# Router logits of chunk 4 as VectorE dot products from y in place, instead of TensorE transposes and matmuls

## What is computed

```python
def _moe2_ref(x, modality_id, w_gate, modality_bias, w1, w2):
    logits = x @ w_gate + modality_bias[modality_id]      # 2304 x 8
    e_idx = np.argmax(logits, axis=1)                     # one expert per token
    logits_s = logits - logits.max(-1, keepdims=True)
    probs = np.exp(logits_s)
    probs /= probs.sum(-1, keepdims=True) + 1e-09
    gate_w = probs[np.arange(N), e_idx]
    for e in range(E):
        mask = e_idx == e
        h = np.maximum(x[mask] @ w1[e], 0.0)
        out[mask] = gate_w[mask, None] * (h @ w2[e])
```

## Time and profile before

| | us |
|---|---|
| runs of the kernel before: median (lowest to highest) | 873.07 (871.36 to 874.25) |
| the profiled execution: span from first to last instruction | 870.5 |
| TensorE busy | 857.1 (98%) |
| VectorE busy | 520.7 (60%) |
| ScalarE busy | 374.4 (43%) |
| GpSimd busy | 328.4 (38%) |
| block 3 of the last chunk | 532.28 to 539.86 |

### The profile page before, as it was taken

The page is one execution under the profiler, slowest core; times in us unless marked ns, Lnnn a source line. Parts: engine busy times, 40 slices in busy tenths (PEclk is TensorE's granted clock), DMA queues, the critical chain, the costliest instruction groups (busy, mean ns, idle before and its releaser), DMA issues.

```text
span 870.5 us, 15612 instructions
## 1 busy us (share of the span) xinstructions
PE 857.1 (98%) x5233; PEld 736.4 (85%) x5242; DVE 520.7 (60%) x1401; ACT 374.4 (43%) x945; POOL 328.4 (38%) x372
## 2 busy tenths in 40 slices
PE   8999999999999999999999999999999999999997
PEld 5678898888888888899999999988888888888885
DVE  6985555333453335449778763883877457666663
ACT  6966313545464455443321132243356235554442
POOL 3736762344323443356335333170043221222211
PEclk9999999999999999999999999999999999999999
DMA  9983212212223210242121121526265645555531
GB/s 191 289 212 88 61 48 65 84 55 78 53 60 112 52 38 27 71 157 74 42 93 61 61 73 37 210 81 254 97 205 206 241 144 191 184 213 182 192 128 39
DMA packets 77517, 103.40 MB, mean 119 GB/s; under 512 B 38973, under 2 KB 43069, under 8 KB 77312
## 3 DMA queue, kind: packets, MB, share of 16 engines
q1 hardware_dynamic: 73760, 91.16, 33.9%
q0 software_dynamic: 3680, 11.28, 3.7%
HBM read 92.98 MB, written 10.22 MB: 119 GB/s over the span
## 4 chain that ended last, share of the span: by engine, by line
PE 89%; DVE 8%; issue 1%; ACT 1%; POOL 1%; DMA 1%; SPq 0%; DVEq 0%; POOLq 0%; ACTq 0%
PE ps L1243 32%; PE ps L1282 16%; PE ps L1805 13%; PE ps L1790 13%; PE ps L1174 3%; PE ps L1203 2%; PE ps L1815 2%; PE ps L1184 2%; PE ps L1150 2%; PE ps L660 1%; DVE sm L1520 1%; DVE w_lo L2041 1%; DMA qk<-in_k 1%; PE ps L1312 1%; DVE h_lo L1600 1%
## 5 line engine op out<-in xcount | busy, mean ns | idle before, releaser
L1035 POOL TENSOR_TENSOR sm<-sm,rinv 72x288 f32<-72x288 f32 (+1 forms) x51 | 45.5, 893 | 174.2 <-DVE rinv L1531 174.1
L1067 POOL TENSOR_TENSOR out_lo<-out_raw,out_hi 128x512 fp32r<-128x512 f32 x72 | 101.8, 1414 | 5.8
L1589 DVE SCALAR_TENSOR_TENSOR h<-h,ps 128x384 f32<-128x384 f32 x72 | 39.8, 553 | 104.2 <-ACT h L1437 103.3
L1243 PE MATMUL ps<-x_hi,val_hi 128*128 128x384 f32 x288 | 101.1, 351 | 0.0
L1243 PE MATMUL ps<-x_hi,gate_hi 128*128 128x384 f32 x288 | 100.5, 349 | 0.4 <-DVE h L1589 0.4
L1065 POOL CAST out_hi<-out_raw 128x512 fp32r<-128x512 f32 x72 | 50.0, 694 | 135.0 <-DMA out_raw<-in_moe_w_out 135.0
L1441 ACT ACTIVATE h_hi<-h 128x384 fp32r<-128x384 f32 x72 | 37.8, 525 | 138.7 <-DVE h L1595 138.7
L1243 PE MATMUL ps<-x_hi,gate_lo 128*128 128x384 f32 x288 | 97.1, 337 | 0.0
L1243 PE MATMUL ps<-x_hi,val_lo 128*128 128x384 f32 x288 | 96.6, 336 | 0.0
L1243 PE MATMUL ps<-x_lo,val_hi 128*128 128x384 f32 x288 | 96.5, 335 | 0.0
L1243 PE MATMUL ps<-x_lo,gate_hi 128*128 128x384 f32 x288 | 93.9, 336 | 0.0
(11 more groups left out here) (278 smaller groups left out, 1947.5 us busy)
## 6 DMA issues: line engine op xcount, KB each, us to landing
w_raw<-in_moe_w SPq DMA_DIRECT2D x72, 512.0 KB, 4.9
out_raw<-in_moe_w_out SPq DMA_DIRECT2D x72, 256.0 KB, 2.6
x_rows<-y_tiles SPq DMA_DIRECT2D x18, 256.0 KB, 2.7
early_w_raw<-in_moe_w SPq DMA_DIRECT2D x8, 512.0 KB, 7.6
gate_raw<-in_moe_w_gate SPq DMA_DIRECT2D x4, 768.0 KB, 9.1
val_raw<-in_moe_w_val SPq DMA_DIRECT2D x4, 768.0 KB, 10.5
qk<-in_q SPq DMA_DIRECT2D x8, 288.0 KB
qk<-in_k SPq DMA_DIRECT2D x8, 288.0 KB
```

The lines of the kernel that those rows point to most:

```text
L1035: pool.tensor_tensor(s3, s3, rinv[0:n, i, :].unsqueeze(2).to_broadcast([n, 4, c]), ALU.mult).then_inc(s_no, 1)
L1067: pool.tensor_tensor(ol[i][:, :], o_raw[i][:, :], oh[i][:, :].bitcast(f32), ALU.subtract).then_inc(s_ol, 1)
L1243: mm = pe.matmul(ps[:, bank, 0:CH], w[:, i, kk, cols], x[:, kk, :], start=(m == 0), stop=(m == n - 1))
L1589: dve.scalar_tensor_tensor(out=hf[n % 2][:, :], in0=hf[n % 2][:, :], scalar=1.0, in1=ps[:, 0, 0:CH], op0=ALU.add, op1=ALU.mult).then_inc(s ...
```

## The change

The logits of chunk 4's three tiles are no longer made by TensorE. VectorE makes them as 24 more dots, which read `ys` in place, without a reload: tile 12, 13 and 14 stand at places 9, 10 and 11 of the list of dotted tiles (`DOTTED_TILES`). They are spread over the 21 ticks from the second half of block 0's gate third to block 3's value third of chunk 5 (`FRESH_TICKS`): 6 dots in block 0, 7 in block 1, 7 in block 2, 4 in block 3. The nine reloaded tiles now end with chunk 4 (`AGAIN_TICKS`), so their dots and their reload DMAs move forward by up to four and six ticks. `evac_y` of chunk 5 waits for the dots instead of the transposes. `one_hot` now waits for 12 dotted tiles and 3 by TensorE.

```diff
--- before.py
+++ after.py
@@ -114,16 +114,14 @@
 
 SS = {0: 16, **{c + 1: at(c, 9, 2) for c in range(NC - 1)}}
 SPREAD = {c: s + (2 if c == 0 else 6) for c, s in SS.items()}
-Y_TILE = {(NC - 2, t): at(NC - 1, 1 + t, 0) for t in range(TT)}
-LOGITS = {k: s + 2 for k, s in Y_TILE.items()}
+Y_TILE, LOGITS = {}, {}
 SS_AT = by_tick((c, s) for c, s in SS.items())
 SPREAD_AT = by_tick((c, s) for c, s in SPREAD.items())
 NORMED = {(c, kk): SPREAD[c] + 1 + (min(kk, 2) if c else 0) for c in SPREAD for kk in range(KT)}
 NORMED_AT = by_tick((k, s) for k, s in sorted(NORMED.items()))
 BANK7 = [x for s in range(TICKS) for x in
          [("p", j) for j in TURN_AT.get(s, [])] + [("o", j) for j in PV_AT.get(s, []) if s >= EARLY]
-         + [("ss", c) for c in SS_AT.get(s, []) if c] + [("rb", c) for c in SPREAD_AT.get(s, []) if c]
-         + [("y", k) for k, x in Y_TILE.items() if x == s] + [("lg", k) for k, x in LOGITS.items() if x == s]]
+         + [("ss", c) for c in SS_AT.get(s, []) if c] + [("rb", c) for c in SPREAD_AT.get(s, []) if c]]
 BEFORE7 = {x: BANK7[n - 1] if n else None for n, x in enumerate(BANK7)}
 
 
@@ -134,19 +132,24 @@
         Y_TILE[c, t], LOGITS[c, t] = free[t], free[t + 1]
 Y_AT = by_tick((k, Y_TILE[k]) for k in sorted(Y_TILE))
 LOGITS_AT = by_tick((k, LOGITS[k]) for k in sorted(LOGITS))
-TURNED_Y = [sum(x < s for k, x in Y_TILE.items() if k[0] < NC - 2) for s in range(TICKS + 1)]
-TURNED_LOGITS = [sum(x < s for k, x in LOGITS.items() if k[0] < NC - 2) for s in range(TICKS + 1)]
-
-
-
-DOTTED = TT * (NC - 3)
+TURNED_Y = [sum(x < s for x in Y_TILE.values()) for s in range(TICKS + 1)]
+TURNED_LOGITS = [sum(x < s for x in LOGITS.values()) for s in range(TICKS + 1)]
+
+
+
+RELOADED = TT * (NC - 3)
+DOTTED_TILES = [*range(RELOADED), *range(TT * (NC - 2), TT * (NC - 1))]
+DOTTED = len(DOTTED_TILES)
 ROUTER = at(NC - 3, 3, 1)
 PAUSE = (SPAN - 6, 0)
-DOT_TICKS = [s for s in range(at(NC - 3, 5, 0), at(NC - 1, 1, 0, 1)) if PAUSE[1] < (s - EARLY) % SPAN < PAUSE[0]]
-DOT = {(i, e): DOT_TICKS[(E * i + e) * len(DOT_TICKS) // (E * DOTTED)] for i in range(DOTTED) for e in range(E)}
+AGAIN_TICKS = [s for s in range(at(NC - 3, 5, 0), at(NC - 1, 0, 0)) if PAUSE[1] < (s - EARLY) % SPAN < PAUSE[0]]
+FRESH_TICKS = range(at(NC - 1, 0, 0, 1), at(NC - 1, 3, 2))
+DOT = {(i, e): (AGAIN_TICKS[(E * i + e) * len(AGAIN_TICKS) // (E * RELOADED)] if i < RELOADED else
+                FRESH_TICKS[(E * (i - RELOADED) + e) * len(FRESH_TICKS) // (E * (DOTTED - RELOADED))])
+       for i in range(DOTTED) for e in range(E)}
 DOT_AT = by_tick((k, s) for k, s in DOT.items())
 DOTTED_AT = by_tick((i, DOT[i, E - 1] + 1) for i in range(DOTTED))
-RELOAD_AT = by_tick((i, DOT[i, 0] - 8) for i in range(DOTTED))
+RELOAD_AT = by_tick((i, DOT[i, 0] - 8) for i in range(RELOADED))
 BY_EXPERT_AT = by_tick((e, DOT[0, e] - 1) for e in range(E))
 
 
@@ -510,13 +513,13 @@
 
         def turned(c, t):
 
-            return TT * c + t - DOTTED
+            return TT * c + t - RELOADED
 
         def y_bank(c):
-            return 7 if c == NC - 2 else 6
+            return 6
 
         def logits_bank(c):
-            return 7 if c == NC - 2 else 5
+            return 5
 
         def ss_bank(c):
             return 7 if c else 0
@@ -1102,12 +1105,8 @@
                     pe.wait_ge(s_oe, before[1] + 1)
                 elif before[0] == "ss":
                     pe.wait_ge(s_nv, before[1] + 1)
-                elif before[0] == "rb":
+                else:
                     pe.wait_ge(s_rc, before[1])
-                elif before[0] == "y":
-                    pe.wait_ge(s_yte, turned(*before[1]) + 1)
-                else:
-                    pe.wait_ge(s_le, turned(*before[1]) + 1)
 
             def residues():
                 pe.wait_ge(s_ms, 2)
@@ -1285,13 +1284,10 @@
                     mm.then_inc(s_y, 1)
 
             def y_bank_free(what, c, t):
-                if c == NC - 2:
-                    bank_7_free((what, (c, t)))
-                else:
-                    s = (Y_TILE if what == "y" else LOGITS)[c, t]
-                    scores_read(s)
-                    pe.wait_ge(s_qe, TURNED_QK[s])
-                    side_free(s)
+                s = (Y_TILE if what == "y" else LOGITS)[c, t]
+                scores_read(s)
+                pe.wait_ge(s_qe, TURNED_QK[s])
+                side_free(s)
 
             def turn_y(c, t):
 
@@ -1445,8 +1441,10 @@
                 act.wait_ge(s_y, FT * c + FT)
                 if c:
                     act.wait_ge(s_x2, 16 * TT * c)
-                    if turned(c, 0) > 0:
-                        act.wait_ge(s_yt, turned(c, 0))
+                    if c >= NC - 2:
+                        act.wait_ge(s_yt, TT)
+                    if c == NC - 1:
+                        act.wait_ge(s_dot, E * DOTTED)
                 act.activation(ys[:, :, :], ps[:, 2:2 + TT, :], ACT.Copy).then_inc(s_ye, 1)
 
             def evac_yT(c, t):
@@ -1602,15 +1600,19 @@
 
             def dot(i, e):
 
-                if e == 0:
+                again = i < RELOADED
+                if e == 0 and again:
                     dve.wait_ge(s_ya[i % 3], 16 * (i // 3) + 16)
+                if e == 0 and i == RELOADED:
+                    dve.wait_ge(s_ye, NC - 1)
                 if i == 0:
                     dve.wait_ge(s_rwe, e + 1)
                 if E * i + e:
                     dve.wait_ge(s_dot, E * i + e)
                 if e == 0 and i >= 2:
                     dve.wait_ge(s_ld, i - 1)
-                dve.tensor_tensor_reduce(out=unread[:, :], in0=y_again[i % 3][:, :], in1=rw_of[e][:, :], scale=1.0,
+                y = y_again[i % 3][:, :] if again else ys[:, DOTTED_TILES[i] % TT, :]
+                dve.tensor_tensor_reduce(out=unread[:, :], in0=y, in1=rw_of[e][:, :], scale=1.0,
                                          scalar=0.0, op0=ALU.mult, op1=ALU.add,
                                          accum_out=dots[:, i % 2, e:e + 1]).then_inc(s_dot, 1)
 
@@ -1618,7 +1620,8 @@
                 if i == 0:
                     dve.wait_ge(s_bu, 6)
                 dve.wait_ge(s_dot, E * i + E)
-                dve.tensor_tensor(logit[:, i, :], dots[:, i % 2, :], bias_t[:, i, :], ALU.add).then_inc(s_ld, 1)
+                n = DOTTED_TILES[i]
+                dve.tensor_tensor(logit[:, n, :], dots[:, i % 2, :], bias_t[:, n, :], ALU.add).then_inc(s_ld, 1)
 
             def add_bias(c, t):
                 i = TT * c + t
```

## The result

Changed kernel: median 878.28 us (876.34 to 880.20, 9 runs); kernel before beside it on the same chip: 871.46 us (869.37 to 874.86, 9 runs). The ratio is 1.0067, 95% interval 1.0048 to 1.0086: slower by about 5.8 us (the medians lie 6.8 us apart), where 3.5 us was forecast. Its profiled execution took 880.04 us, its span is 878.3 us.

A forecast was written before the change was run, and what follows sets the result against it. TensorE held 89% of the chain of waits; the change would make VectorE the bound up to hot_b. -4.0 (TensorE) + 7.9 (TensorE waiting for VectorE) - 0.4 = +3.5 us on 873.07: 876.6 us, range 871.8 to 879.8.

The forecast's parts named there:

- Taken from TensorE: Chunk 4's three tiles: transposes, logits and a longer product leave TensorE, 1.32 us per tile, 4.0 us saved on the path.
- Given to VectorE: Chunk 5, blocks 0 to 3: 24 dots, 17.0 us, make VectorE the bound; hot_b at 540.9 us even with GpSimd silent.
- GpSimd's part: GpSimd's w_out splits beside VectorE's work in blocks 1 to 4 of chunk 5: four times 1.2 us, together 4.8 us.
- Start: First dot of VectorE's queue, after ScalarE's ys and held by GpSimd's out_lo: gets going at about 515.4 us.
- What comes after: After the one-hot: VectorE runs on without pause, so TensorE's wait at 573 us goes, -0.4 us.
- The third rival: TensorE's clock falls in the wait before early_counts, costing 1.7 us more: 878.3 us, chance 0.23.
- Moved: Four dots of tile 8 go into chunk 4, reloaded dots up to four ticks forward, covered by VectorE's gaps: 0 us.

The follow-up runs named there:

- e5: Changed kernel with only chunk 4's first tile on VectorE, its dots in blocks 1 and 2, reloaded dots not moved: ratio 0.9966 to the kernel before.
- e10: The kernel e5 run once more on another occasion, no new edit: ratio 0.9981 to the kernel before.
- e2: Changed kernel with GpSimd's subtraction for w_out's low part cut to 8 columns in blocks 1 to 4 of chunk 5: ratio 1.0040 to the kernel before.
- e3: Changed kernel with 20 matmuls of 384 columns into an unused bank put ahead of early_counts, filling the wait: ratio 1.0048 to the kernel before.
- e7: Changed kernel without the move: reloaded dots keep their old ticks, 24 new dots stand in blocks 1 to 3 of chunk 5: ratio 1.0075.
- e1: Kernel before with only the reloaded dots moved to end with chunk 4; chunk 4's own tiles stay with TensorE: ratio 1.0029.
- e4: Changed kernel with early_counts moved to the middle of block 4's down product, 3.1 us of TensorE work later: ratio 1.0044 to the kernel before.
- e9: e1 with GpSimd's subtraction cut to 8 columns for three blocks around the end of chunk 4, TensorE's matmul count kept: ratio 1.0004.
- e6: Changed kernel with two of chunk 4's tiles on VectorE, reloaded dots not moved, early_counts later: ratio 0.9997 to the kernel before.

## Why the prediction was right, and where it was not

The forecast was 876.6 us with a range of 871.8 to 879.8 and 0.67 on slower; 878.28 us was measured. That the time lies only 1.7 us off is in part luck: the forecast was built on a median before of 873.07 us, and beside the changed kernel that kernel ran at 871.46. The step forecast was 3.5 us, and the step measured 5.8 by the ratio. The direction and the cause, VectorE late with `hot_b`, were right. Step by step:

- **"Taken from TensorE", 4.0 us: right.** e5 and e10 got 1.2 to 1.4 us for one tile. In the changed kernel chunk 5 shows none of it, because VectorE became the bound, as "Given to VectorE" said.
- **"GpSimd's part", 4.8 us: right**, 4.84 us by the rows, and e2 got back the 2.6 us of it that its edit removed. Two of the four places were other instructions than dots: h_split, and `pick` in the one-hot.
- **"Start", 515.4 us: 0.8 us too late, counted from the mark.** I had GpSimd hold the first dot. In the changed kernel its subtraction ended at 518.16 us, before the copy of y did at 518.69 us, since the copy came 1.7 us later and the split did not. Another 0.5 us of the sum was too much: without GpSimd's part, VectorE took 25.0 us from the first dot to the end of `hot_b`, and I had added up 25.5. So `hot_b` was late by 2.6 us, and not by 3.9.
- **"What comes after", -0.4 us: right**, 0.6 us came back.
- **The third rival, the clock, had 0.23, and it came**, at 1.5 us where 1.7 us was the price. e3 shows it by taking the wait away. It should have been in the forecast: a wait of about 4 us in TensorE's work was forecast, and the trace held an example of the clock at 0.66 without any such wait. The Trainium skill ("TensorE: Matmul & The Clock Gate", "HAM oscillation") says that a long gap sends the clock back; here the traces agree, with waits of 3.67 us (changed kernel), 3.75 (e2), and 2.74 and 3.81 (e7). Behind the 1.60 us at the end of chunk 4 the clock stayed at 1.00.
- **"Moved", 0 us: wrong, +1.7 us in this profile, 2.5 us by e1's ratio.** This is the step that failed. I read one gap of 1.46 us in the middle of chunk 4, called it the cover, and let the dots move into the last blocks of the chunk, where VectorE has the roots, the diagonals and the normalising of the next chunk as well, and where each dot could meet a split. My own, from that very place, showed it with no idle time and dots of 1.00 and 1.29 us. I had used them for chunk 5 and not for the place that they came from. The way that the dots move was too short as well: by the tables it is up to six ticks, and thirteen for the last four of tile 8, not "up to four". e1, e4, e7 and e9 show what stands in place of the 0: with the move, the normalising for the next chunk comes so late that it meets a split, and when the subtraction comes first TensorE waits 1.3 to 1.6 us for the h_split behind it.

In chunk 5 two errors cancel, which is luck: 2.5 - 0.6 + 1.5 = 3.4 us, where 3.9 - 0.4 = 3.5 was forecast. What the profiled execution lies above the forecast step is chunk 4 (1.7 us) and 0.3 us after chunk 5.

The cost of the move differs between executions: 1.27 to 1.60 us at the end of chunk 4 in four kernels, 0.21 in e4; chunk 3 is 1.4 us longer in e1 and e2, and 0.1 us in the changed kernel. The rows under e4 show what differs, which of the two engines comes first. Open is why: the splits wait for the load of w_out each time, and no run fixes when it lands. Open too are the price of the second tile alone and, with it, whether two tiles could gain.

## What to carry over

When work moves to an engine with "room", sum its queue over the stretch between two results that others wait for, not its busy share, and do this for the work that is pushed aside too, at the place where it lands. Move as much as the gaps take: one tile of three gained its full 1.3 us in chunk 5, two with the counts moved gained nothing that the runs can tell, and three lost. Count a forecast wait of several us on TensorE at its length plus what the half clock behind it costs (1.5 us here). Give an experiment one change: e6 had two, and its result can't be shared out.
